# Hidden rows of a mixture of experts through DRAM and VectorE transposes instead of TensorE transposes

## The chip, the cores and the metric

The kernel runs on one core of one Trainium2 chip. The metric is the time of one execution in microseconds (us), as the device records it, with all inputs and the output in the chip's memory (DRAM). Lower is better. TensorE is called PE in the rows, VectorE DVE, ScalarE ACT, GpSimd POOL and SyncE SP.

## What is computed

Three stages follow each other: attention with a sliding window and four sink keys, a dense layer, and a mixture of eight experts. The change lies in the third stage alone, on 1536 tokens of 512 numbers:

```python
# x: 1536 x 512, w1: 8 x 512 x 1024, w2: 8 x 1024 x 512
logits = x @ w_gate
noisy_logits = logits + np.log1p(np.exp(x @ w_noise)) * noise
top2 = the two largest of each row of noisy_logits
top2_w = softmax over these two
for e in range(8):
    for k in range(2):
        mask = top2[:, k] == e
        h = np.maximum(x[mask] @ w1[e], 0.0)
        out[mask] += top2_w[mask, k, None] * (h @ w2[e])
```

All matrix products are of fp32 accuracy: an operand is split in a rounded part ("hi", in the matmul type fp32r) and the rest ("lo"), and three products (hi by hi, hi by lo, lo by hi) are summed.

## The kernel before

The five engines run programs written by hand, with an explicit semaphore for each hand-over; an engine's instructions run in the order of its code. A buffer number behind a name tells copies apart; `bank0` to `bank7` are the eight PSUM banks.

**Sorting.** After the dense layer each token's row is scattered to `sorted_x` in DRAM, grouped by expert. The experts' rows are then cut into tiles of 128 rows; there are `TILES` = 31 slots for tiles, and this input fills 29 of them (tiles 29 and 30 are computed for nothing). Tables made by VectorE (`tile_row_i`, `tile_expert_i`, `tile_slot_i`, `tile_end_i`) say where each tile's rows lie, whose expert they are, which half of the weight ring they use, and after which tile each expert ends. By the requests for weights in the trace the first six experts end behind tiles 3, 7, 10, 14, 17 and 20.

**One tile** is five steps. `turn_rows(t)`: TensorE transposes the tile's rows `xs` (4 transposes into bank 0), and ScalarE and VectorE copy them out as `xsT_hi` and `xsT_lo` (`rows_turned_out`). `up(t)`: 24 matmuls with the first matrix into banks 1 and 2. `relu_out(t)`: ScalarE and VectorE write one half each of `hid`, 128 rows by 1024. `turn_hidden(t)`: TensorE transposes `hid` (8 transposes into banks 3 and 4), and the two engines copy them out as `hidT_hi` and `hidT_lo` (`hid_turned_out`). `down(t)`: 24 matmuls with the second matrix into bank 5; VectorE copies the result to `ys` (`result_out`) and ScalarE's queue stores it to `sorted_y` in DRAM (`store_rows`).

**Order on TensorE.** The loop over tiles 3 to 29 has the order of these lines, so the second matrix lags one tile behind the first:

```python
with pe.Fori(3, TILES - 1) as t:
    up(t)
    turn_rows(t + 1)
    down(t - 1)
    turn_hidden(t)
```

**Between tiles 2 and 3** VectorE also computes the gates, ten small instructions (lines 1212 to 1220); in the changed kernel they stand behind its first two transposes, and the turned rows of tile 4 and the ReLU of tile 3 behind them.

**Weights.** The ring has two halves of 8 MB, one expert each. An expert's 4 MB come as four pieces of 1 MB into `ring_raw` (pieces 0 and 1 the first matrix, 2 and 3 the second), and GpSimd splits each in place into hi and lo (`split`, two instructions a piece). From the third expert on GpSimd's own queue requests the pieces, all four when `expert_done` says that the expert two before has ended. SyncE's queue loads the tiles' rows.

**End.** When all real tiles are stored, GpSimd gathers each token's second row (`gathered_b`, 12 indirect transfers), VectorE weighs and adds it, and SyncE stores the output.

Below are the functions that the diff touches.

## Time and profile before

| | |
|---|---|
| Time, median of 3 runs (lowest, highest) | 782.83 us (780.29, 783.93) |
| The profiled execution | 780.96 us |
| Its span, first to last instruction | 779.3 us |
| Mean granted TensorE clock, as a share of full speed | 0.991 |
| Busy share of PE, DVE, ACT, POOL | 97%, 38%, 29%, 58% |

The profile is of one execution; the times in its rows are in us from the first instruction. The device's time of that execution is 1.66 us more than the span. An engine that is busy for most of the span need not be the one that sets the end; that is read from the chain of work that ended last.

### The profile page before, as it was taken

What the parts mean: (1) busy time and instruction counts of PE and PEld (TensorE: products, weight loads), DVE (VectorE), ACT (ScalarE), POOL (GpSimd) and SP (SyncE); (2) the same over time, 40 slices, a digit from 0 to 9 for tenths busy, and PEclk for the clock granted to TensorE, in tenths of its full rate; (3) what the DMA queues carried; (4) which work ended last, traced back from release to release, by engine and by line L of the source; (5) the groups of instructions that cost most, each with busy time, mean ns of one, the idle gap of its engine ahead of it and who ended that gap; (6) DMA issues with size and microseconds to landing.
All of it is one profiled execution on the core that took longest, in us unless ns stands there. A gap on an engine that the chain in (4) does not pass through costs nothing.

```text
span 779.3 us, 13024 instructions
## 1 busy us (share of the span) xinstructions
PE 758.5 (97%) x4116; PEld 640.3 (82%) x4117; DVE 298.1 (38%) x821; ACT 225.9 (29%) x527; POOL 454.2 (58%) x264
## 2 busy tenths in 40 slices
PE   7999999999999999999999999999999999999993
PEld 5677889899989999898877888888888888888882
DVE  4777543235323522444564222223222222322225
ACT  5999522233223222322412111111111111111110
POOL 6888996000300200049699395798939898954723
PEclk8999999999999999999999999999999999999998
DMA  8642493000200100043631431617143434315228
GB/s 287 235 138 91 143 341 118 0 2 0 82 1 0 52 28 0 0 156 124 259 122 55 150 146 41 256 40 257 52 167 130 159 137 167 130 53 161 82 79 285
DMA packets 37276, 92.06 MB, mean 118 GB/s; under 512 B 5761, under 2 KB 5889, under 8 KB 37249
## 3 DMA queue, kind: packets, MB, share of 16 engines
q1 hardware_dynamic: 22416, 45.83, 16.9%
q0 software_dynamic: 10368, 37.75, 13.4%
q10 hardware_dynamic: 4464, 8.13, 2.8%
q8 instruction: 15, 0.25, 0.1%
q14 instruction: 13, 0.10, 0.0%
HBM read 67.06 MB, written 24.64 MB: 118 GB/s over the span
## 4 chain that ended last, share of the span: by engine, by line
PE 93%; DMA 2%; POOL 2%; ACT 1%; issue 1%; DVE 1%; POOLq 0%; ACTq 0%; DVEq 0%
PE bank L1465 21%; PE bank L1493 21%; PE bank L1379 17%; PE bank L1329 17%; PE bank L1282 4%; PE bank L1273 3%; PE bank L1474 3%; PE bank L1255 2%; DMA gathered_b<-sorted_y,arena 2%; PE bank L1454 2%; PE bank L1395 1%; POOL gathered_b L715 1%; PE bank L1389 1%; ACT arena L739 1%; POOL arena L643 0%
## 5 line engine op out<-in xcount | busy, mean ns | idle before, releaser
L1493 PE MATMUL bank<-ring,hidT_hi 128*128 (+1 forms) x496 | 158.4, 400 | 2.2 <-DVE hidT_lo L1114 2.2
L621 POOL TENSOR_TENSOR ring<-ring_raw,ring 128x2048 fp32r<-128x2048 f32 x32 | 148.0, 4625 | 2.5
L667 POOL DMA_INDIRECT sorted_x<-y_rows,arena x24 | 25.2, 1050 | 204.5 <-DVEq L1049 198.4
L1465 PE MATMUL bank<-ring,xsT_hi 128*128 (+1 forms) x496 | 136.0, 396 | 1.5 <-DVE xsT_lo L1096 1.5
L619 POOL TENSOR_TENSOR ring<-ring_raw,ones 128x2048 fp32r<-128x2048 f32 x32 | 115.8, 3619 | 22.1 <-DMA ring_raw<-in_moe_w 22.1
L1379 PE MATMUL bank<-w_out_sb,gated_hi 128*128 128x512 f32 x384 | 121.2, 397 | 0.0
L1493 PEld LDWEIGHTS bank<-ring,hidT_hi 128*128 128x128 f32 x496 | 90.9, 188 | 22.5 <-issue 2.7
L1465 PEld LDWEIGHTS bank<-ring,xsT_hi 128*128 128x128 f32 x496 | 90.9, 188 | 19.6 <-issue 2.2
L1493 PE MATMUL bank<-ring,hidT_lo 128*128 (+1 forms) x248 | 97.9, 395 | 0.0
L1329 PE MATMUL bank<-xT_hi,w_in_hi 128*128 (+1 forms) x256 | 86.8, 339 | 0.0
L1329 PE MATMUL bank<-xT_lo,w_in_hi 128*128 (+1 forms) x256 | 86.1, 336 | 0.0
L1329 PE MATMUL bank<-xT_hi,w_in_lo 128*128 (+1 forms) x256 | 86.0, 336 | 0.0
L1379 PEld LDWEIGHTS bank<-w_out_sb,gated_hi 128*128 128x128 f32 x384 | 71.2, 188 | 12.5
L970 DVE TENSOR_TENSOR arena<-bank,arena 128x384 f32<-128x384 f32 x64 | 35.6, 557 | 114.7 <-ACT arena L794 110.6
L854 ACT CAST hidT_hi<-bank 128x512 fp32r<-128x512 f32 x62 | 33.3, 590 | 156.8 <-PE bank L1474 156.8
L1465 PE MATMUL bank<-ring,xsT_lo 128*128 (+1 forms) x248 | 76.6, 390 | 0.0
L1379 PE MATMUL bank<-w_out_sb,gated_lo 128*128 128x512 f32 x192 | 76.0, 396 | 0.0
L794 ACT ACTIVATE arena<-bank 128x384 f32<-128x384 f32 x64 | 31.4, 491 | 138.9 <-PE bank L1329 138.9
L1108 DVE COPY ys<-bank 128x512 f32<-128x512 f32 x30 | 20.8, 692 | 122.5 <-PE bank L1493 122.5
L1101 DVE TENSOR_SCALAR hid<-bank 128x512 f32<-128x512 f32 x31 | 21.4, 691 | 114.5 <-PE bank L1465 114.5
L849 ACT ACTIVATE hid<-bank 128x512 f32<-128x512 f32 x31 | 18.5, 598 | 151.6 <-PE bank L1465 151.6
L974 DVE TENSOR_TENSOR gated_lo<-arena,gated_hi 128x384 fp32r<-128x384 f32 x64 | 44.6, 697 | 40.4 <-ACT gated_hi L799 40.4
(184 smaller groups left out, 1093.8 us busy)
## 6 DMA issues: line engine op xcount, KB each, us to landing
ring_raw<-in_moe_w POOLq DMA_DIRECT2D x24, 1024.0 KB, 9.3
ring_raw<-in_moe_w SPq DMA_DIRECT2D x8, 1024.0 KB, 6.3
xs<-sorted_x SPq DMA_DIRECT2D x31, 256.0 KB
sorted_y<-ys ACTq DMA_DIRECT2D x31, 256.0 KB
sorted_y<-zeros SPq DMA_DIRECT2D x1, 4864.0 KB, 25.1
arena<-in_k SPq DMA_DIRECT2D x8, 520.0 KB, 4.1
w_in_raw<-in_moe_w_in SPq DMA_DIRECT2D x2, 2048.0 KB, 9.4
arena<-in_q SPq DMA_DIRECT2D x8, 384.0 KB, 3.2
```

The lines of the kernel that those rows point to most:

```text
L619: pool.tensor_tensor(hi, raw, one_like(raw), ALU.mult).then_inc(rounded, 1)
L621: ins = pool.tensor_tensor(lo, raw, hi.bitcast(F32), ALU.subtract)
L667: pool.indirect_dma_start(out=sorted_x[:, :], out_offset=bass.IndirectOffsetOnAxis(ap=row_at[k][:, kk:kk + 1], axis=0), in_=y_rows_all[:, ...
L794: act.activation(tanh_h[fc % 2][:, :], bank[fc % 2][:, 0:BLK], ACT.Tanh).then_inc(tanh_ready, 1)
L854: act.copy(hidT_hi[:, half * BANK:(half + 1) * BANK], bank[3 + half][:, :]).then_inc(hidT_rounded, 1)
L970: dve.tensor_tensor(gated[fc % 2][:, :], bank[fc % 2][:, 0:BLK], tanh_h[fc % 2][:, :], ALU.subtract).then_inc(gated_ready, 1)
L974: dve.tensor_tensor(gated_lo[fc % G][:, :], gated[fc % 2][:, :], gated_hi[fc % G][:, :].bitcast(F32), ALU.subtract).then_inc(gated_split, 1)
L1282: last = pe.matmul(attn_bank[half][D * u:D * u + D, at:at + w], lhs, rhs, start=start, stop=stop, skip_group_check=True)
L1329: last = pe.matmul(bank[fc % 2][:, 0:BLK], w[:, at:at + P], x[:, bass.ds(blk * CH + c, 1), :].rearrange("p a s -> p (a s)"), start=c == 0 ...
L1379: last = pe.matmul(bank[2 + kk][:, :], g[fc % G][:, kk * P:(kk + 1) * P], w_out_sb[:, fc, w, :], start=fc == 0 and n == 0, stop=fc == FC - ...
L1465: last = pe.matmul(bank[1 + half][:, :], x[:, c * P:(c + 1) * P], ring[:, bass.ds(at * 2 * WE + (w + c * FE + half * BANK), BANK)], start= ...
L1493: last = pe.matmul(bank[5][:, :], x[:, c * P:(c + 1) * P], ring[:, bass.ds(at * 2 * WE + (w + CH * FE + c * DM), DM)], start=c == 0 and n ...
```

## The change

For tiles 2 to 30 `hid` is no longer transposed by TensorE. ScalarE's queue writes it to a DRAM tensor `hid_by_lane` (pieces of 1 KB, cut in four column blocks of 256), and reads it back into `hid_lanes`, where partition 32b + i holds rows 4i to 4i+3 of column block b (4 KB that lie together in DRAM). VectorE then transposes blocks of 32 by 32, in two instructions a tile, into the same banks 3 and 4: it reads `hid_lanes` with a step of 8 elements and writes the bank with a step of 4. What follows (`hid_turned_out`) is as before. For the hidden columns to come out in this order, the second matrix is loaded with row 8p + c in partition p, chunk c; tiles 0 and 1 are still transposed by TensorE, whose transposes therefore read `hid` with a step of 8 columns.

The second matrix now lags two tiles: while `down(t - 2)` runs, the rows of tile t travel. `up` waits in addition until banks 1 and 2 are evicted (`evicted`). The loads of tile rows move from SyncE's queue to ScalarE's from tile 4 on. SyncE's queue requests the weights from the third expert on: the first matrix once the expert two before has had its last `up`, the second once it has had its last `down`.

```diff
-        xsT_hi = place_at("xsT_hi", xsT_at, [DM], F32R)
-        xsT_lo = place_at("xsT_lo", xsT_at + DM, [DM], F32R)
+        xsT_hi = [place_at(f"xsT_hi{b}", xsT_at + 2 * b * DM, [DM], F32R) for b in range(2)]
+        xsT_lo = [place_at(f"xsT_lo{b}", xsT_at + (2 * b + 1) * DM, [DM], F32R) for b in range(2)]
...
+        hid_cols = hid[:, :].rearrange("p (r c) -> p c r", c=EC)
+        lane_blocks = hid_lanes[:, :].rearrange("p (g r c) -> p g c r", g=QUAD, c=EC)
...
+        hid_by_lane = nc.dram_tensor("hid_by_lane", (QUAD, P, FE // QUAD), F32, kind="Internal").ap()
...
-        w2_view = w2.rearrange("e (c o p) n -> p (e c) o n", o=2, p=P)
+        w2_view = w2.rearrange("e (p c o) n -> (e p) c o n", o=2, p=P)
...
+            for e in range(RING, E):
+                expert = expert_at(e)
+                last = sp.value_load(tile_end_i[0:1, e - RING:e - RING + 1], min_val=1, max_val=TILES)
+                for j, (used_up, n) in enumerate(((hid_ready, last), (hid_ready, last),
+                                                  (expert_done, last + 1), (expert_done, last + 1))):
+
+                    sp.wait_ge(used_up, n)
+                    dst, src = raw_piece(e, expert, j)
+                    sp.dma_start(dst, src).then_inc(piece_loaded[e % RING][j], 16)
...
-                    for j in range(4):
-                        dst, src = raw_piece(e, expert, j)
-                        pool.dma_start(dst, src).then_inc(piece_loaded[j], 16)
...
+            def load_rows(t):
+
+                act.wait_ge(xs_turned, t)
+                at = act.value_load(tile_row_i[0:1, bass.ds(t, 1)], min_val=0, max_val=E * CAP - P)
+                act.dma_start(xs[:, :], sorted_x[bass.ds(at, P), :]).then_inc(xs_loaded, 16)
+
+            def hid_out(t, first=False):
+
+                act.wait_ge(relu_act, t + 1)
+                act.wait_ge(relu_dve, t + 1)
+                if not first:
+
+                    act.wait_ge(hid_read, 16 * (t - 2))
+                act.dma_start(hid_by_lane.rearrange("b t q -> t b q"),
+                              hid[:, :].rearrange("t (b q) -> t b q", b=QUAD)).then_inc(hid_written, 16)
+
+            def hid_in(t, first=False):
+                act.wait_ge(hid_written, 16 * (t - 1))
+                if not first:
+
+                    act.wait_ge(hid_turned, 2 * t)
+                act.dma_start(hid_lanes[:, :], hid_by_lane.rearrange("b (i g) q -> (b i) (g q)", g=QUAD)
+                              ).then_inc(hid_read, 16)
...
+            def tile(t, load=True):
+                relu_out(t)
+                hid_out(t)
+                rows_turned_out(t + 1)
+                if load:
+                    load_rows(t + 2)
+                hid_in(t)
+                hid_turned_out(t - 1, used=t)
+                store_rows(t - 2)
...
+            def turn_hidden(t):
+
+                dve.wait_ge(hid_read, 16 * (t - 1))
+                for half in range(2):
+
+                    dve.wait_ge(hidT_ready, 2 * t - 1 + half)
+                    dve.transpose(bank[3 + half][:, :].rearrange("p (c i g) -> p g c i", c=EC // 2, g=QUAD),
+                                  lane_blocks[:, :, half * (EC // 2):(half + 1) * (EC // 2), :]).then_inc(hid_turned, 1)
...
+            def tile(t):
+                relu_out(t, written=True)
+                rows_turned_out(t + 1)
+                result_out(t - 2)
+                hid_turned_out(t - 1)
+                turn_hidden(t)
...
             pe.wait_ge(tables_ready, 1)
-            up(2)
-            turn_rows(3)
-            turn_hidden(2)
-            with pe.Fori(3, TILES - 1) as t:
-                up(t)
+            up(2, rows=3)
+            up(3, b=1, evicted=True, rows=4)
+            with pe.Fori(4, TILES - 1) as t:
+                up(t, evicted=True)
                 turn_rows(t + 1)
-                down(t - 1)
-                turn_hidden(t)
-            up(TILES - 1)
+                down(t - 2)
+            down(TILES - 3)
+            up(TILES - 1, evicted=True)
             down(TILES - 2)
-            turn_hidden(TILES - 1)
             down(TILES - 1)
```

VectorE, the loop over tiles, of before: one round is the ReLU of the right half (`hid`), the rest of the turned rows (`xsT_lo`), the result (`ys`), and the two halves of `hidT_lo`.

```order
L1231 ISA
L1101 TENSOR_SCALAR hid_86<-bank2 128x512
L1095 REGISTER_ALU
L1096 TENSOR_TENSOR xsT_lo_88<-bank0,xsT_hi_87 128x512
L1107 ISA
L1108 COPY ys_84<-bank5 128x512
L1113 ISA
L1114 TENSOR_TENSOR hidT_lo_83<-bank3,hidT_hi_82 128x512
L1113 REGISTER_ALU
L1114 TENSOR_TENSOR hidT_lo_83<-bank4,hidT_hi_82 128x512
```

The same loop of the changed kernel, from the turned rows on; the ReLU stands just ahead of these rows.

```order
L1144 TENSOR_TENSOR xsT_lo0_89<-bank0,xsT_hi0_87 128x512
L1168 COPY ys_84<-bank5 128x512
L1173 ISA
L1174 TENSOR_TENSOR hidT_lo_83<-bank3,hidT_hi_82 128x512
L1173 REGISTER_ALU
L1174 TENSOR_TENSOR hidT_lo_83<-bank4,hidT_hi_82 128x512
L1149 REGISTER_ALU
L1152 ISA
L1153 STREAM_TRANSPOSE bank3<-hid_lanes_91 128x4x128
L1153 STREAM_TRANSPOSE bank4<-hid_lanes_91 128x4x128
L1296 REGISTER_ALU
L1296 COMPARE_AND_BRANCH
```

Two transposes stand last in the round, so the next tile's ReLU stands behind them.

ScalarE, the loop over tiles, of before: ReLU of the left half, the turned rows, the two halves of `hidT_hi`, and the request to store `ys`.

```order
L849 ACTIVATE hid_86<-bank1 128x512
L844 REGISTER_ALU
L845 CAST xsT_hi_87<-bank0 128x512
L853 ISA
L854 CAST hidT_hi_82<-bank3 128x512
L853 REGISTER_ALU
L854 CAST hidT_hi_82<-bank4 128x512
L858 ISA
L858 DMA sorted_y<-ys_84 128x512
```

The same loop of the changed kernel, behind the ReLU and up to the first half of `hidT_hi`.

```order
L860 DMA hid_by_lane<-hid_86 128x4x256
L844 REGISTER_ALU
L845 CAST xsT_hi0_87<-bank0 128x512
L850 ISA
L850 TENSOR_LOAD arena_75
L850 ISA x2
L851 ISA
L851 DMA xs_85<-sorted_x 128x512
L864 ISA
L867 REGISTER_ALU
L868 DMA hid_lanes_91<-hid_by_lane 128x1024
L880 ISA
```

Three requests have come in between: the write of `hid`, the load of the rows of tile t + 2, and the read into `hid_lanes`, which waits for the write and stands ahead of the copies to `hidT_hi`.

## Rows read from the trace of the kernel before

**Rows 1.** The page: span, then busy time, share and instructions of each engine.

```profile
span 779.3 us, 13024 instructions
...
PE 758.5 (97%) x4116; PEld 640.3 (82%) x4117; DVE 298.1 (38%) x821; ACT 225.9 (29%) x527; POOL 454.2 (58%) x264
```

**Rows 2.** The chain that ended last, from 390 us: start, length, what.

```profile
405.84 5.46 PE bank L1465 x24
...
411.32 0.60 ACT hid L849
...
414.04 5.74 PE bank L1465 x24
...
426.67 5.48 PE bank L1465 x24
432.15 0.44 PE bank L1454 x4
432.59 5.60 PE bank L1493 x24
438.19 0.88 PE bank L1474 x8
...
637.27 5.71 PE bank L1465 x24
...
736.60 5.47 PE bank L1465 x24
742.07 0.44 PE bank L1454 x4
742.50 5.60 PE bank L1493 x24
...
749.17 2.04 DMA sorted_y<-ys
...
751.97 0.99 POOL gathered_b L715
...
776.13 0.75 DVE gathered_a L1239
```

**Rows 3.** Two tiles' stretches: busy by engine, clock, DMA share, GB/s.

```profile
426.67:439.06 12.39, 12.39 (x62) 10.23 (x61) 3.36 (x5) 2.15 (x5) 2.80 (x2) 1.00 0.14 42
439.06:451.46 12.40, 12.40 (x62) 10.23 (x61) 3.37 (x5) 2.15 (x5) 8.32 (x6) 1.00 0.88 323
```

**Rows 4.** Groups by line: busy us, mean ns, idle before.

```profile
L1114 DVE TENSOR_TENSOR hidT_lo<-bank,hidT_hi 128x512 fp32r<-128x512 f32 x62 | 39.9, 686 | 8.1 <-ACT hidT_hi L854 7.7 <-issue 0.4
...
L1474 PE MATMUL bank<-ident,hid 128*128 128x128 f32 x248 | 32.2, 273 | 0.3 <-ACT hid L849 0.3
...
L621 POOL TENSOR_TENSOR w_out_sb<-w_out_raw,w_out_sb 128x512 fp32r<-128x512 f32 x16 | 21.7, 1354 | 1.3
...
L1101 DVE TENSOR_SCALAR hid<-bank 128x512 f32<-128x512 f32 x31 | 21.4, 691 | 114.5 <-PE bank L1465 114.5
```

**Rows 5.** DMA issues: count, KB each, median us from issue to landing.

```profile
ring_raw<-in_moe_w POOLq DMA_DIRECT2D x24, 1024.0 KB, 9.3
...
arena<-in_k SPq DMA_DIRECT2D x8, 520.0 KB, 4.1
...
arena<-in_q SPq DMA_DIRECT2D x8, 384.0 KB, 3.2
```

**Rows 6.** VectorE in order of time, the gates behind tile 2, first and last.

```profile
414.49 0.16 DVE L1212 TENSOR_SCALAR bank<-arena 128x12 f32<-128x12 f32 x1
...
416.02 0.17 DVE L1220 TENSOR_TENSOR arena<-arena,bank 128x12 f32<-128x12 f32 x1
```

**Rows 7.** GpSimd in order of time: request of the seventh expert, splits of its first matrix.

```profile
614.94 2.97 POOL L696 DMA_DIRECT2D ring_raw<-in_moe_w  x4
620.47 3.60 POOL L619 TENSOR_TENSOR ring<-ring_raw,ones 128x2048 fp32r<-128x2048 f32 x1 [2.56 <-DMA ring_raw<-in_moe_w]
...
632.39 4.61 POOL L621 TENSOR_TENSOR ring<-ring_raw,ring 128x2048 fp32r<-128x2048 f32 x1
```

More of the change, by code:

```diff
@@ L436, in raw_piece @@
             else:
[L437 removed]
+                src = w2_view[bass.ds(expert * P, P), :, j - 2, :]
             return piece(ring_raw[e % RING], j), src
@@ L555, in _ @@
             sp.wait_ge(tile_rows_known, 1)
-            with sp.Fori(2, TILES) as t:
-                start = tile_start(t)
-                sp.wait_ge(scattered, 16 * TOP * TT)
+            sp.wait_ge(scattered, 16 * TOP * TT)
+            for t in (2, 3):
                 sp.wait_ge(xs_turned, t)
-                load_rows(start)
+                load_rows(sp.value_load(tile_row_i[0:1, t:t + 1], min_val=0, max_val=E * CAP - P))
+            sp.wait_ge(tables_ready, 1)
+            for e in range(RING, E):
[6 more added lines that the diff above has]
+                    sp.dma_start(dst, src).then_inc(piece_loaded[e % RING][j], 16)
             for i in range(TT):
@@ L849, in relu_out, with hid_turned_out @@
                 act.activation(hid[:, 0:BANK], bank[1][:, :], ACT.Relu).then_inc(relu_act, 1)
-            def hid_turned_out(t):
+            def hid_turned_out(t, used=None):
+                if used is not None:
+                    act.wait_ge(expert_done, used)
                 for half in range(2):
@@ L870, in _ @@
             act.activation(gate_e[:, :], gate_d[:, :], ACT.Exp).then_inc(route_act, 1)
-            def tile(t, more):
-                relu_out(t)
-                if more:
-                    rows_turned_out(t + 1)
-                hid_turned_out(t)
-                store_rows(t - 1)
             relu_out(1)
@@ L883, in _ @@
             store_rows(1)
+            rows_turned_out(3, 1)
+            act.wait_ge(tile_rows_known, 1)
+            act.wait_ge(scattered, 16 * TOP * TT)
+            load_rows(4)
             relu_out(2)
-            rows_turned_out(3)
-            hid_turned_out(2)
-            with act.Fori(3, TILES - 1) as t:
-                tile(t, True)
-            tile(TILES - 1, False)
+            hid_out(2, first=True)
+            hid_in(2, first=True)
+            rows_turned_out(4)
+            load_rows(5)
+            relu_out(3)
+            hid_out(3)
+            hid_turned_out(2, used=3)
+            hid_in(3)
+            def tile(t, load=True):
[7 more added lines that the diff above has]
+                store_rows(t - 2)
+            with act.Fori(4, TILES - 2) as t:
+                tile(t)
+            tile(TILES - 2, load=False)
+            store_rows(TILES - 3)
+            hid_turned_out(TILES - 2, used=TILES - 1)
+            relu_out(TILES - 1)
+            hid_out(TILES - 1)
+            hid_in(TILES - 1)
+            hid_turned_out(TILES - 1, used=TILES)
+            store_rows(TILES - 2)
             act.wait_ge(expert_done, TILES + 1)
@@ L1205, in _ @@
             result_out(1)
+            rows_turned_out(3, 1)
             relu_out(2)
-            rows_turned_out(3)
-            hid_turned_out(2)
+            turn_hidden(2)
             dve.wait_ge(route_act, 3 * NBLK + 1)
@@ L1221, in _ @@
             dve.sem_inc(gates_ready, 1)
-            def tile(t, more):
-                relu_out(t)
-                if more:
-                    rows_turned_out(t + 1)
-                result_out(t - 1)
-                hid_turned_out(t)
-            with dve.Fori(3, TILES - 1) as t:
-                tile(t, True)
-            tile(TILES - 1, False)
+            rows_turned_out(4)
+            relu_out(3, written=True)
+            hid_turned_out(2)
+            turn_hidden(3)
+            def tile(t):
[4 more added lines that the diff above has]
+                turn_hidden(t)
+            with dve.Fori(4, TILES - 1) as t:
+                tile(t)
+            result_out(TILES - 3)
+            hid_turned_out(TILES - 2)
+            relu_out(TILES - 1, written=True)
+            turn_hidden(TILES - 1)
+            result_out(TILES - 2)
+            hid_turned_out(TILES - 1)
             for i in range(TT):
@@ L1461, in up @@
                 pe.wait_ge(xsT_ready, t + 1)
+                if evicted:
+                    pe.wait_ge(relu_act, t)
+                    pe.wait_ge(relu_dve, t)
                 for c in range(CH):
-                    for n, (x, w) in enumerate(((xsT_hi, 0), (xsT_hi, WE), (xsT_lo, 0))):
+                    if rows is not None and c == CH // 2:
+                        turn_rows(rows)
+                    for n, (x, w) in enumerate(((xsT_hi[b], 0), (xsT_hi[b], WE), (xsT_lo[b], 0))):
                         for half in range(2):
```

48 lines of the change are left out of this document (21 added, 27 removed).

## The prediction, on record before the changed kernel ran

> **What bounds the kernel now.** I read the page first. TensorE is busy for 97% of the span, and the next, GpSimd, for 58% [rows 1]. Then the chain that ended last, in order of time, from tile 2 to the end [rows 2]. From 426.67 us it is TensorE alone: `up` 5.48 us, `turn_rows` 0.44, `down` 5.60, `turn_hidden` 0.88, and then the next `up` at 439.06, without a gap. The two tile stretches say the same: PE is busy for all of 12.39 us, while VectorE works 3.36 and ScalarE 2.15, at full clock, whether no weights travel (42 GB/s) or four pieces do (323 GB/s) [rows 3]. So a tile costs what TensorE is given, and the other engines have over 8 us to spare in each. The second thing to see is the end: the chain leaves TensorE when `down(28)`, begun at 742.50, is done; its result is stored, the gathers begin at 751.97, and the rest of the 779.3 us is gathers and stores [rows 2]. Tiles 29 and 30 run beside them.
>
> **The sum** is made in the span of the profiled execution, 779.3 us.
>
> *TensorE's transposes.* From the start of `up(4)` at 426.67 to the end of `up(29)` at 742.07 there are 25 whole tiles and one `up` [rows 2]. Each whole tile loses its 8 transposes, 0.88 us: 12.39 becomes 11.51. That is 25 x 0.88 = **-22.0 us**, if nothing else is late.
>
> *What must hide.* The rows now take this way: ReLU, ScalarE's request, write to DRAM, ScalarE's request, read back, two VectorE transposes, and only then VectorE's next ReLU, which stands behind them in its program. This is a ring of one round per tile, so a tile can't be shorter than the ring. Its parts:
> - ReLU 0.69 [rows 4].
> - The write of 512 KB. Below: the 256 KB store of `ys` landed in 2.04 us [rows 2]. Above: 520 KB of keys in 4.1 [rows 5], which shared the queues with other loads. I take 3.2, between them, since pieces of 1 KB to DRAM have no row.
> - The read of 512 KB. Below: 384 KB in 3.2; above again 4.1 [rows 5]. I take 3.8, by size.
> - The two transposes. The trace has none. Below: 0.65 each, as the other 128x512 instructions of VectorE, which run at 0.686 and overlap a little; above: 1.35, GpSimd's subtraction of that size [rows 4]. No step of 8 elements in a big VectorE instruction is in the trace either. I take 0.65, since the work is one pass over as many elements, so 1.3.
> - Three hand-overs of 0.1.
>
> That is 0.69 + 3.2 + 3.8 + 1.3 + 0.3 = 9.3 us against 11.51, with bounds 7.5 (2.04 + 3.2 + 1.3 + 1.0) and 11.9 (4.1 + 4.1 + 2.7 + 1.0). Moreover the ReLU may end up to some 5.3 us after `up` without TensorE noticing, as `turn_rows` and `down` (6.04) come before the next `up`, and `xsT_lo` (0.69) stands behind the ReLU; it now ends 0.7 after. So 4.6 us of lateness can be borrowed. The work itself has room: VectorE 3.36 + 1.3 = 4.7 of 11.51, ScalarE 2.15 and four requests, of about 0.4 each.
>
> *The Trainium skill* (DMA: Bandwidth & Descriptors, section "Anatomy of one DMA") gives 2.0 us and bytes/436e3 for a transfer on GpSimd's path, so 3.2 us for each leg by estimate. The ring would be 8.7 and the start below 0.6 shorter. No row here has a lone 512 KB transfer.
>
> *Weights.* The requests leave GpSimd (2.97 us per expert [rows 7]) and come apart: the first matrix about a tile earlier, the second about one later. Each pair of pieces is 2 MB, 6 us at 323 GB/s [rows 3], beside the write or the read. If it doubles a leg, each costs 3 to 4 us of the ring; two per expert make up to 7, against 3 to 4 tiles with 2.2 us to spare in each, and 4.6 borrowed. I take 0. GpSimd itself was at its limit once: it requested the seventh expert at 614.94, split the first matrix from 620.47 to 637.00 [rows 7], and the `up` that needs it ran from 637.27 for 5.71 instead of 5.48 [rows 2]. Now, with `up(4)` at 424.7, `up(14)` ends at 545 and `down(14)` at 574, which releases the sixth expert's second matrix; it lands 6 us later and is split by 597, and the seventh's first matrix, long loaded, is split by 613; `up(21)` wants it at 620. So 7 us to spare, and no wait.
>
> *The start.* `up(2)` starts at 405.84 as before and holds the 4 transposes of the rows: it ends at 411.75. `up(3)` must now wait for the ReLU: 412.5, and ends with its own 0.44 at 418.4. `down(2)` no longer fills the time behind it, and `up(4)` waits for VectorE: 412.5 + 7.3 (legs and hand-overs) = 419.8, transposes 421.1, the gates, 1.7 us from 414.49 to 416.19 [rows 6], 422.8, `xsT_lo` and ReLU 424.2; the second request of weights falls in the read, +0.5: 424.7. Before it was 426.67. The work of `down(2)` and `turn_hidden(3)` is thus displaced, not lost: **-2.0 us**. With legs of 5.2 in all it would be -3.8, with the upper bounds +0.6.
>
> *The end.* `down(28)` used to follow `up(29)` by 0.44. Now `down(27)` is between, 5.60, and since `hidT` is one buffer, `down(28)` also waits for ScalarE's and VectorE's first half: 0.6 + 0.7 + 0.1 = 1.4. **+7.0 us**. What queues behind on VectorE, `result_out(28)`, stands behind `turn_hidden(29)`, which by the ring ends 3 us before `down(28)`.
>
> *Gathers* now share the DMA engines with the write and read of tile 30, 1 MB against 6 MB of gathers and stores: **+0.5 us** (0 to 2). TensorE's 16 transposes with a step of 8, tiles 0 and 1: 0 to 1.8 (twice their 0.88 each), mostly beside other waits; I take 0.
>
> Sum: -22.0 - 2.0 + 7.0 + 0.5 = -16.5. Span 762.8, its own time 764.5 instead of 780.96. The median before is 1.87 us above that execution, so I take the difference from the median: 782.83 - 16.5 = **766.3 us**, -2.1%.
>
> **Rivals.** A measurement of this kernel can hardly tell 0.5%, 3.9 us, from no change: 778.9 to 786.7.
>
> - *The ring is a little short of hidden* (0.15): bursts of weights or legs of 4.1 us use up the borrowed 4.6, and TensorE waits a few us at each of six experts. With 1 to 2 us each, 772 to 779.
> - *The gain is eaten* (0.10): 779 to 787. It needs a ring of about 12.2 us: 25 x (12.2 - 11.5) + 2.9 at the start - 4.6 borrowed = 16.
> - *The legs through DRAM are slow and the kernel gets slower* (0.10): the write and read together over 9.9 us instead of 7.0. At 10.7 the ring is 13.0: 766.3 + 25 x 1.5 + 3.7 - 4.6 = 803. For it: 1 KB pieces, the weights, two transfers of rows on the same queue. Against: 42 GB/s in most stretches [rows 3], and 4.1 us for 520 KB with neighbours.
> - *The transposes are slow* (0.08): over 2.1 us each, the ring again passes 12.2. At 2.4 each it is 12.8: 766.3 + 32 + 3.5 - 4.6 = 797. For it only the steps of 8 read and 4 written; against it, no row of VectorE above GpSimd's 1.35 us for this size. The Trainium skill (SBUF — State Buffer, section "Door 1") says that each access to a new 16-byte line pays, and that PSUM's lines have 8 bytes; these steps leave the line at each element. It gives no price for VectorE.
>
> **How the numbers follow.** The forecast, 761 to 772, has 0.57. Below it the shortest ring gives -1.8 more at the start, the gathers may cost nothing (-0.5), and the medians scatter by 2 to 3: low 761. Above, I go through the eaten gain and the edge of the slower cases: high 789, which leaves out the worst of them. Faster is the forecast and the first rival, 0.72; same 0.10; slower 0.18.
>
> **What would show it.** `turn_hidden`'s pieces gone from the chain, and tiles of 11.51 us on TensorE. The transposes near 0.65 us each, the write and read near 3.2 and 3.8. `up(4)` starting 12.2 us after `up(3)` did, behind a wait for VectorE's ReLU. A wait of 1.4 us ahead of `down(28)`, and gathers from about 735. GpSimd idle more often, for weights. If instead each `up` waits for VectorE's ReLU and VectorE for `hid_lanes`, the ring is the bound and I am wrong; if TensorE waits for `ring`, it is the weights.

## The result, and the profile after

The changed kernel took 789.26 us (median of 7 runs, 786.34 to 792.28) against 783.59 for the kernel before (median of 7, 780.29 to 784.06): the ratio is 1.0079, with a 95% interval from 1.0056 to 1.0103. It is slower by 0.8%, where 2.1% less was forecast. The profiled execution took 789.29 us, its span is 787.4.

The page of the changed kernel, with the rows that answer to [rows 1, 4, 5]:

```profile
span 787.4 us, 12786 instructions
...
PE 746.5 (95%) x3884; PEld 624.8 (79%) x3885; DVE 358.1 (45%) x879; ACT 229.1 (29%) x528; POOL 436.4 (55%) x240
...
L1153 DVE STREAM_TRANSPOSE bank<-hid_lanes 128x512 f32<-128x512 f32 x58 | 64.0, 1148 | 44.5 <-DMA hid_lanes<-hid_by_lane 44.5
...
ring_raw<-in_moe_w SPq DMA_DIRECT2D x32, 1024.0 KB, 8.4
hid_by_lane<-hid ACTq DMA_DIRECT2D x29, 512.0 KB, 3.1
hid_lanes<-hid_by_lane ACTq DMA_DIRECT2D x29, 512.0 KB, 3.4
```

TensorE is busy for 12 us less than before, although 29 tiles no longer have their transposes of 0.88 us: matmuls that run slower behind pauses, below, take the rest. The median write and read are as fast as assumed. But the span is 8 us longer: TensorE stands still for some 20 us more. The chain that ended last shows where (start, length, what):

```profile
412.80 3.25 DMA hid_by_lane<-hid
416.07 3.42 DMA hid_lanes<-hid_by_lane
419.51 2.10 DVE bank L1153 x2
...
424.89 8.50 PE bank L1542 x24
433.39 0.44 PE bank L1524 x4
433.83 5.59 PE bank L1571 x24
439.43 5.44 PE bank L1542 x24
...
450.90 5.44 PE bank L1542 x24
...
468.81 8.63 DMA hid_by_lane<-hid
...
504.85 10.37 DMA hid_by_lane<-hid
515.32 0.33 ACTq L868
...
519.53 7.40 PE bank L1571 x24
...
592.12 11.22 DMA hid_by_lane<-hid
...
721.76 5.46 PE bank L1542 x24
...
747.06 7.39 PE bank L1571 x24
```

The tile from 439.43 to 450.90 takes 11.47 us, as forecast (12.39 in [rows 2, 3]). Then, at five of the six loads of a first matrix, the chain leaves TensorE for a *write* of `hid` that takes 8.5 to 11.2 us; with nothing else under way a write takes 2.9 to 3.3 (two more slow ones, 8.54 at 556.32 and 10.28 at 632.19, aren't shown). Behind each TensorE starts late, and where it stood still longest the next 24 matmuls take 7.4 us instead of 5.6. What is asked for around the write at 504.85, in order of time, first on SyncE's queue (two views, the second a part of the first), then on ScalarE:

```profile
498.59 6.44 SPq L577 DMA_DIRECT2D ring_raw<-in_moe_w  x4
...
504.05 0.99 SPq L577 DMA_DIRECT2D ring_raw<-in_moe_w  x2
```

```profile
503.90 0.60 ACT L873 ACTIVATE hid<-bank 128x512 f32<-128x512 f32 x1 [4.29 <-PE bank L1542]
504.85 0.38 ACTq L860 DMA_DIRECT2D hid_by_lane<-hid  x1
...
515.32 0.33 ACTq L868 DMA_DIRECT2D hid_lanes<-hid_by_lane  x1
515.77 0.59 ACT L881 CAST hidT_hi<-bank 128x512 fp32r<-128x512 f32 x1 [9.85 <-DMA hid_by_lane<-hid]
```

The end of an expert's last `up` releases both the request for the next first matrix (2 MB, at 504.05) and, one ReLU later, the write (at 504.85). Of the four requests in the first row, the two at 498.59 and 499.35 are the second matrix of the expert before; it landed only at 509.86. So this write has 4 MB beside it. It is the same at the writes of 11.22 and 10.28 us. At the two of 8.63 and 8.54 us only the 2 MB of the first matrix were under way, and at the one load that is left, the first in time (419.52), the write came 5.2 us behind the request and took 3.75. ScalarE can ask for the read only when the write has landed, and the copies to `hidT_hi`, which the next `down` needs and which have nothing to do with this transfer, stand behind that request. The waits of the whole span (us in total, times, longest):

```profile
ACT hidT_hi L881 <- DMA hid_by_lane<-hid: 57.8, 9, 10.7
...
PE bank L1571 <- DVE hidT_lo L1174: 13.7, 6, 7.3
```

ScalarE's wait is this large in total. But of TensorE's 13.7 us for `hidT_lo` only 3.0, in three waits, fall between 430 and 725 us, where the collisions are; the rest is at the end of the kernel. So the late copies alone don't explain the loss.

There is a second victim. ScalarE's load of the next tile's rows, asked for at 506.19, lands just as late (median 2.8 us, longest 10.7). TensorE in order of time:

```profile
516.74 0.66 PE L1524 MATMUL bank<-ident,xs 128*128 128x128 f32 x4 [1.41 <-DMA xs<-sorted_x]
519.53 1.22 PE L1571 MATMUL bank<-ring,hidT_hi 128*128 x2 [2.14 <-issue]
```

`turn_rows` waits 1.41 us for `xs`, and the `down` behind it starts 2.14 later, though its first half of `hidT_lo` was done at 517.07. What fills the 2.14 us is in TensorE's own program: between `turn_rows` and `down` it reads two registers (lines 1557 and 1558, the tile's expert and its half of the ring). Such a read took 0.30 to 1.18 us. In a quiet tile both are done while `up` still runs; here they stand behind the wait for `xs`, at 516.85 and 518.47. So it is at all five collisions:

| `xs` landed | first half of `hidT_lo` done | `down` starts |
|---|---|---|
| 478.03 | 479.29 | 480.47 |
| 516.69 | 517.08 | 519.53 |
| 565.44 | 566.72 | 567.71 |
| 604.13 | 605.19 | 606.90 |
| 643.05 | 644.32 | 645.51 |

`down` starts 1.0 to 2.5 us after its data are there and 2.3 to 2.8 us after `xs` has landed, so `xs` with the two reads behind it is what releases it. The matmuls themselves stood still for `xs` at three of the five (1.41, 1.57 and 0.43 us). The share of each victim is an estimate: at the three big collisions TensorE stood still for 9.4 us, and with `xs` on time the copies alone would have left some 5 of it, from the end of an undisturbed `turn_rows` to the time in the second column. At the two small ones (0.73 and 0.47 us ahead of `down`) they would have left nothing; there some 0.3 and 0.4 us came ahead of the next `up` as well, by the way that was forecast: write, read, transposes, VectorE's ReLU.

Four stretches with the columns of [rows 3]; first the tile of `up(4)` and a quiet one, then the wait and the `down` behind it:

```profile
424.89:439.43 14.54, 14.54 (x53) 11.66 (x54) 4.85 (x6) 2.26 (x4) 14.38 (x5) 0.80 0.46 167
439.43:450.90 11.47, 11.47 (x53) 9.38 (x53) 5.58 (x7) 2.26 (x4) 6.64 (x2) 1.00 0.48 158
...
510.00:519.53 9.53, 5.99 (x28) 4.51 (x27) 2.04 (x4) 1.64 (x3) 9.37 (x4) 1.00 0.83 304
519.53:526.93 7.40, 7.40 (x25) 5.95 (x26) 3.29 (x4) 0.59 (x1) 7.40 (x2) 0.77 0.43 122
```

The clock granted to TensorE is 0.80 and 0.77 in the stretches that follow a pause, so it stood at the lower level, 1.2 GHz, for part of them; before the first of the two TensorE had been idle for 5.57 us (from 419.32), before the other for 1.41 and 2.14.

### The profile page after: what moved, and what is told of

Its sections match the earlier page's. It is cut to its first block, busy times and chain, and to the rows that moved or that the text cites. A ratio compares the mean times of both kernels' runs of the same rounds, so it can differ in the third digit from the quotient of the medians.

```text
span 787.4 us, 12786 instructions
## 1 busy us (share of the span) xinstructions
PE 746.5 (95%) x3884; PEld 624.8 (79%) x3885; DVE 358.1 (45%) x879; ACT 229.1 (29%) x528; POOL 436.4 (55%) x240
## 4 chain that ended last, share of the span: by engine, by line
PE 80%; DMA 11%; DVE 3%; issue 2%; ACT 2%; POOL 1%; ACTq 0%; DVEq 0%; POOLq 0%
PE bank L1449 17%; PE bank L1399 17%; PE bank L1542 17%; PE bank L1571 16%; DMA hid_by_lane<-hid 8%; PE bank L1352 4%; PE bank L1343 3%; DMA hid_lanes<-hid_by_lane 3%; PE bank L1325 2%; PE bank L1465 1%; DVE bank L1153 1%; DVE hid L1161 1%; PE bank L1524 1%; PE bank L1459 1%; ACT arena L739 1%
## 5 line engine op out<-in xcount | busy, mean ns | idle before, releaser
L1571 PE MATMUL bank<-ring,hidT_hi 128*128 (+1 forms) x496 | 165.1, 415 | 17.9 <-DVE hidT_lo L1174 13.7
L1571 PEld LDWEIGHTS bank<-ring,hidT_hi 128*128 128x128 f32 x496 | 95.3, 197 | 41.4 <-issue 20.0
L1542 PEld LDWEIGHTS bank<-ring,xsT_hi 128*128 128x128 f32 x496 | 94.0, 191 | 29.2 <-issue 9.5
L1571 PE MATMUL bank<-ring,hidT_lo 128*128 (+1 forms) x248 | 101.2, 408 | 0.0
L1153 DVE STREAM_TRANSPOSE bank<-hid_lanes 128x512 f32<-128x512 f32 x58 | 64.0, 1148 | 44.5 <-DMA hid_lanes<-hid_by_lane 44.5
L1571 PEld LDWEIGHTS bank<-ring,hidT_lo 128*128 128x128 f32 x248 | 48.7, 197 | 12.0
L1174 DVE TENSOR_TENSOR hidT_lo<-bank,hidT_hi 128x512 fp32r<-128x512 f32 x62 | 39.9, 685 | 33.9 <-ACT hidT_hi L881 33.7
```

The lines of the kernel that those rows point to most:

```text
L1153: dve.transpose(bank[3 + half][:, :].rearrange("p (c i g) -> p g c i", c=EC // 2, g=QUAD), lane_blocks[:, :, half * (EC // 2):(half + 1) * ...
L1174: dve.tensor_tensor(hidT_lo[:, cols], bank[3 + half][:, :], hidT_hi[:, cols].bitcast(F32), ALU.subtract).then_inc(hidT_ready, 1)
L1542: last = pe.matmul(bank[1 + half][:, :], x[:, c * P:(c + 1) * P], ring[:, bass.ds(at * 2 * WE + (w + c * FE + half * BANK), BANK)], start= ...
L1571: last = pe.matmul(bank[5][:, :], x[:, c * P:(c + 1) * P], ring[:, bass.ds(at * 2 * WE + (w + CH * FE + c * DM), DM)], start=c == 0 and n ...
```

## The experiments

**Theory A**: the first matrix's burst meets the write, ScalarE's program makes `down` start late by it, and a late restart costs 2 to 3 us more at the lower clock. No expectation speaks of the load of `xs` in the same burst, and no run moves it alone. **Rivals**: it is the ring as a whole that is too long (slow transposes, slow legs), or the order in ScalarE's program alone. Each diff is against the changed kernel, where no other is named. Each time is a median, each ratio is to the kernel before, which had medians of 781.86 to 782.84 us beside these runs.

### No weights on the way

```diff
-            for e in range(RING, E):
-                ...
-                    sp.dma_start(dst, src).then_inc(piece_loaded[e % RING][j], 16)
...
+                    pool.wait_ge(hid_ready, last + 1)
+                    pool.sem_inc(up_split, 1)
+                    pool.wait_ge(expert_done, last + 2)
+                    pool.sem_inc(down_split, 1)
```

It leaves out the loads and splits of the weights from the third expert on.

> This kernel leaves out the loads and the splits of all experts' weights from the third on (they compute with the first two experts' weights); the rest is as in the changed kernel. Theory A, the write of hid is slow only beside the load of a first matrix: every write takes about 3.1 us as the median one does, no `up` or `down` waits behind `up(4)`, and the time falls by what the tiles from 4 to 28 took over 11.48 us each beyond the slow restart, 18 us, to about 771. Rival B, the way of the rows through DRAM is too long by itself for some tiles, whatever else travels: waits stay and the time is above 783.

Measured: 772.22 us, ratio 0.9874 (0.9855 to 0.9892). Writes and reads between tiles 4 and 27 never stand on the chain; what is left are the first restart (`up(4)` 7.12 us) and the end. So the ring in itself is short enough, the rival "the whole ring is too long" falls, and the 16 to 17 us (by the ratios, by the medians) come from the weights. By this run alone that could also be their splits; the next one moves only a request.

### The first matrix requested after the write

```diff
-                for j, (used_up, n) in enumerate(((hid_ready, last), (hid_ready, last),
+                for j, (used_up, n) in enumerate(((moved, last), (moved, last),
...
                 act.wait_ge(hid_written, 16 * (t - 1))
+                act.sem_inc(moved, 1)
```

> SyncE requests an expert's first matrix only once the write of hid of the last tile that used it has landed, about 4 us later than now. Theory A: the four writes of 8.6 to 11.2 us fall to near 3.5, the reads behind them lengthen from 3.4 to some 6 to 8, but nothing on ScalarE waits for a read, so the `down`s no longer wait; about 772 (768 to 778). Rival B: 787 to 790, since the same bytes travel in the same tile. Rival D, the weights become late for GpSimd: TensorE waits for the ring, over 790.

Measured: 771.48 us, ratio 0.9868 (0.9846 to 0.9889): with all the work done it is as fast as without weights. ScalarE and, below, SyncE and VectorE in order of time, for the expert that had the write of 11.22 us:

```profile
584.17 0.38 ACTq L861 DMA_DIRECT2D hid_by_lane<-hid  x1
...
588.66 0.39 ACTq L870 DMA_DIRECT2D hid_lanes<-hid_by_lane  x1
589.32 1.08 ACT L883 CAST hidT_hi<-bank 128x512 fp32r<-128x512 f32 x2 [4.01 <-PE bank L1574]
```

```profile
588.71 0.96 SPq L578 DMA_DIRECT2D ring_raw<-in_moe_w  x2
```

```profile
593.82 2.24 DVE L1156 STREAM_TRANSPOSE bank<-hid_lanes 128x512 f32<-128x512 f32 x2 [2.59 <-DMA hid_lanes<-hid_by_lane]
```

The same burst now starts with the read (0.05 us behind its request), and the read is through in 5.0 us (588.66, and the transposes begin at 593.82). Nothing on ScalarE stands behind the read, and VectorE has the time. The copies wait for TensorE's `down`, as they should. The load of `xs`, asked for at 585.54, is ahead of the burst too, so this edit cures both victims and doesn't weigh them apart.

### The first matrix requested after the read

The same with `moved` counted by VectorE when it has waited for the read.

```diff
                 dve.wait_ge(hid_read, 16 * (t - 1))
+                dve.sem_inc(moved, 1)
```

> SyncE requests an expert's first matrix only once the read into hid_lanes of the last tile that used it has landed, some 7.5 us later than now. Theory A: the burst now falls between a read and the next write, of which it may touch the start; writes of at most 5 us, about 770 (767 to 776), equal to or a little better than after the write. Rival B: no change, 787 to 790. Rival D: weights late, over 790.

Measured: 782.56 us (772.51 to 787.76 in ten runs, the widest spread here), ratio 0.9961 (0.9924 to 0.9998), a miss by 12. The burst of 7 to 8 us, moved 5 us later, reaches into the next tile's write. The chain that ended last:

```profile
516.87 6.56 DMA hid_by_lane<-hid
...
533.61 7.04 DMA hid_lanes<-hid_by_lane
...
617.70 7.64 DMA hid_lanes<-hid_by_lane
```

Of the writes behind a first matrix those on the chain take 6.2 to 6.8 us; reads that are requested 0.8 to 1.3 us behind a second matrix take 7.0 to 7.6. The ring's spare time is gone and stays gone. Apart isn't enough; the burst must end before the next write.

### The read requested behind the copies

```diff
-                hid_in(t)
                 hid_turned_out(t - 1, used=t)
                 store_rows(t - 2)
+                hid_in(t)
```

> ScalarE requests the read into hid_lanes behind the copies to hidT_hi and the store, so its wait for the write no longer stands ahead of them; the weights are requested as in the changed kernel. If the order on ScalarE turns slow writes into waits of `down` (13.7 us of TensorE's waits were for hidT_lo), the waits for hidT_lo go away, but the reads of all tiles start later (7.2 us behind `up` instead of 4) and a write of 10 us still makes the next ReLU late: a part of the 18 us comes back, 776 to 783. If the order does not matter, 787 to 790. If the later reads make the ring too long for all tiles, over 792.

Measured: 793.85 us, ratio 1.0128 (1.0093 to 1.0163). The copies no longer wait, but every read starts later, behind TensorE's `down`, and VectorE waits for it in each round:

```profile
DVE bank L1153 <- DMA hid_lanes<-hid_by_lane: 135.3, 29, 8.5
```

In the changed kernel this wait is 44.5 us in 21. The third of the expected outcomes came, a ring too long for all tiles. So the order in ScalarE's program can't simply be turned: the read's early request is what hides the ring. What the order costs beside the weights this run doesn't show, since it lengthens every tile.

### The weights requested 0.6 us behind the write

As the kernel with `moved` after the write, but counted just behind the write's request.

```diff
                               hid[:, :].rearrange("t (b q) -> t b q", b=QUAD)).then_inc(hid_written, 16)
+                act.sem_inc(moved, 1)
...
                 act.wait_ge(hid_written, 16 * (t - 1))
-                act.sem_inc(moved, 1)
```

> SyncE requests an expert's first matrix once the write of hid of the last tile that used it has been requested (not landed), about 1 us later than in the changed kernel; write and load then run beside each other, the write's bytes first in line. Theory A1, a write behind 2 MB of weights waits for all of them (first come, first served on the DMA engines): writes of at most 5 us and the time of w1_after_write, 769 to 775. Theory A2, the DMA engines take turns between the queues, whoever was first: writes still of 6 to 8 us beside the weights, and a time between, 777 to 786.

Measured: 782.81 us, ratio 1.0010 (0.9986 to 1.0035). The time is the one of theory A2, but most of the writes are those of A1. At the loads behind tiles 3, 7, 14 and 20 the write takes 3.5, 3.4, 3.5 and 4.6 us, where in the changed kernel those of tiles 7, 14 and 20 took 8.6, 8.5 and 10.3. So to be first by 0.6 us did protect the write. Only at tiles 10 and 17 it doesn't: 8.8 us (505.99) and 10.1 (589.83, landed by 600.01). There, as at tile 20, the second matrix of the expert before, requested 6.3 us ahead of the write, was still under way. What is asked for behind the weights now pays in the write's place, the read and `xs`:

```profile
554.49 3.45 DMA hid_by_lane<-hid
...
558.04 8.21 DMA hid_lanes<-hid_by_lane
...
591.17 10.62 DMA xs<-sorted_x
```

### Pieces of 4 KB in the write

`hid` goes out in whole rows of 4 KB, and four requests read it back in pieces of 1 KB.

```diff
-                act.dma_start(hid_by_lane.rearrange("b t q -> t b q"),
-                              hid[:, :].rearrange("t (b q) -> t b q", b=QUAD)).then_inc(hid_written, 16)
+                act.dma_start(hid_by_lane[:, :], hid[:, :]).then_inc(hid_written, 16)
...
+                for b in range(QUAD):
+                    act.dma_start(hid_lanes[32 * b:32 * b + 32, :].rearrange("i (g q) -> i g q", g=QUAD),
+                                  hid_by_lane.rearrange("(i g) (b q) -> b i g q", g=QUAD, b=QUAD)[b]
+                                  ).then_inc(hid_read, 16)
```

> The changed kernel with another layout in DRAM: hid is written as whole rows, in pieces of 4 KB, and read back by four requests in pieces of 1 KB; the weights are requested as in the changed kernel. If the write is slow beside the weights because its pieces are small (1 KB against 4 KB of theirs, in turn), it falls from 8.6 to 11.2 us to about 5, and the time to 772 to 778. If it is slow because it stands behind the bytes that are already under way, it stays at 8 or more, and the time at 786 to 794.

Measured: 813.84 us, ratio 1.0384 (1.0336 to 1.0432). A lone write is shorter, 2.63 us; behind a first matrix it takes 4.9 to 8.2, so neither expectation holds as a whole. The moments have moved too: the longest was asked for 1.2 us behind the weights, the others 3 us or more. The time says nothing of the write: the four requests take ScalarE 0.62 us each (median), and the slowest reads beside weights 7.1 to 8.2.

### Pieces of 2 KB and 1 KB in the weights

Two requests of half the columns each, or four of a quarter, for a first matrix; GpSimd waits for all of them.

```diff
+                    if j < 2:
+                        w = FE // 4
+                        for part in range(2 * j, 2 * j + 2):
+                            dst = ring_raw[e % RING][:, 0:2 * PIECE].rearrange("p (c n) -> p c n", c=CH)[:, :, part * w:(part + 1) * w]
+                            src = w1_view[:, bass.ds(expert * CH, CH), part * w:(part + 1) * w]
+                            sp.dma_start(dst, src).then_inc(piece_loaded[e % RING][j], 16)
+                        continue
```

> The changed kernel, but SyncE's two requests for a first matrix take half the columns of all four chunks each, so that their pieces are 2 KB instead of 4 KB; bytes, number and moment of the requests stay. GpSimd waits for both before it splits. Turns by pieces (the write's 512 pieces of 1 KB and the weights' pieces are served alternately, in equal numbers): a lone write is 3.1 us, about 1.4 and 0.5 MB at 300 GB/s; beside 4 KB pieces it ends with all 2.5 MB, 1.4 + 8.3 = 9.7 (8.5 to 11.2 was seen), beside 2 KB pieces when 1.5 MB are through: 1.4 + 5.0 = 6.4 us. Then no `down` is late, the 18 us come back, and the time is 769 to 774. Rival, what is asked first is served first or the bytes alone count: the five writes stay at 8.5 to 11.2 us and the time at 785 to 792.

> As the 2 KB kernel, with four requests of a quarter of the columns each, so pieces of 1 KB. Turns by pieces: the write ends when 1 MB is through, 1.4 + 3.3 = 4.8 us; the weights have 2048 pieces and may themselves take longer than 8.4 us, which GpSimd's splits can bear by some us. Time 769 to 774, as with 2 KB, or up to 3 more if the splits come late. Rival, as before: writes of 8.5 to 11.2 us and 785 to 792.

Measured: 785.04 us, ratio 1.0045 (1.0016 to 1.0073), and 784.01 us, ratio 1.0031 (1.0005 to 1.0056). From the chain of the kernel with 2 KB:

```profile
469.95 8.04 DMA hid_by_lane<-hid
...
505.26 9.25 DMA hid_by_lane<-hid
...
554.54 7.58 DMA hid_by_lane<-hid
```

The five writes have a mean of 8.7 us with 2 KB (7.6 to 9.5) and 8.3 with 1 KB (7.6 to 8.5), against 9.8 in the changed kernel; 6.4 and 4.8 were forecast. Whether the times are better than the changed kernel's isn't clear, since the intervals of the ratios overlap or touch.

The trace also has the start of each piece, and it shows what the forecast left out. With nothing else under way, the first piece of the write starts 0.9 to 1.2 us behind its request. At the five slow writes of the changed kernel it starts 3.6 to 4.0 us behind it, with 1 KB pieces in the weights 3.7 to 4.2. From then on the two queues do take turns by number: from 474 to 475 us the changed kernel started 65 pieces of the write and 70 of the weights (of 4 KB), and from 474.9 to 475.9 the kernel with 1 KB pieces 171 and 200. So turns by number of pieces hold once the write has begun; the 3 us ahead of its first piece, in which only weights move, are what the sum of 4.8 lacked. In the kernel where the write was asked for 0.6 us ahead of the weights, its first piece at tiles 3, 7 and 14 started after 0.9 us, as if alone.

### The order at the start

On the kernel with `moved` after the write. VectorE's ReLU of tile 3 no longer waits behind the transposes of tile 2 and the gates.

```diff
             relu_out(2)
+            rows_turned_out(4)
+            relu_out(3, written=True)
             turn_hidden(2)
+            hid_turned_out(2)
...
-            rows_turned_out(4)
-            relu_out(3, written=True)
-            hid_turned_out(2)
             turn_hidden(3)
```

> On top of w1_after_write (771.5 us), VectorE turns out the rows of tile 4 and does the ReLU of tile 3 ahead of its first two transposes and the gates, not behind them. Theory A says that `up(4)` waits 6.9 us only because VectorE sits in the wait for the first read, and then runs 7.8 us instead of 5.5 at a lower clock: both go away, up(4) starts within 1 us of the end of `up(3)`, and the time falls by 7 to 9 us, to about 763. If the rows' first way through DRAM is the bound instead, the wait moves to `down(2)` and the time stays at 770 to 772.

Measured: 763.67 us, ratio 0.9742 (0.9698 to 0.9787). The chain: `up(3)`, ReLU, `up(4)`.

```profile
419.66 2.79 PE bank L1545 x12
...
422.47 0.70 DVE hid L1164
...
423.42 5.73 PE bank L1545 x24
```

A pause of 1.0 us instead of 7.00 in the kernel it was made from, and `up(4)` takes 5.73 instead of 7.75. (In this execution `up(3)` waited for a split of GpSimd's and started 3 us later than in the other, so the span, 766.7, is longer than the median would have it.)

### Matmuls that keep the clock up

Also on the kernel with `moved` after the write: 27 matmuls into the unused bank 5 fill the pause ahead of `up(4)`.

```diff
             up(3, b=1, evicted=True, rows=4)
+            pe.wait_ge(ys_ready, 2)
+            for _ in range(27):
+                pe.matmul(bank[5][:, :], xsT_hi[1][:, 0:P], xsT_hi[1][:, :], start=True, stop=True)
```

> On top of w1_after_write, TensorE runs 27 matmuls of no use (their result is overwritten) while it waits ahead of up(4), some 6.2 us of work in a wait of 6.9. If the lower clock comes from the idle stretch, `up(4)` takes 5.5 instead of 7.8 us and the time falls by 2.3 us to about 769. If the slow matmuls have another cause, such as a transfer that slows their operands, up(4) stays at 7.8 and the time at 771.

Measured: 769.88 us, ratio 0.9843 (0.9788 to 0.9897). In its chain `up(4)` starts behind as long a wait but takes 5.74 us; without the filler, in the kernel it was made from, 7.75:

```profile
420.92 6.12 PE bank L1602 x27
...
427.13 5.74 PE bank L1545 x24
```

So the 2 us are the clock's and not a wait inside `up`. The time, 1.6 us less, can't be told from 771.48.

### Transposes without steps

Again on the kernel with `moved` after the write: VectorE reads and writes with a step of 1, so the rows come out in another order and the output differs.

```diff
-        lane_blocks = hid_lanes[:, :].rearrange("p (g r c) -> p g c r", g=QUAD, c=EC)
+        lane_blocks = hid_lanes[:, :].rearrange("p (g c r) -> p g c r", g=QUAD, c=EC)
...
-                    dve.transpose(bank[3 + half][:, :].rearrange("p (c i g) -> p g c i", c=EC // 2, g=QUAD),
+                    dve.transpose(bank[3 + half][:, :].rearrange("p (g c i) -> p g c i", c=EC // 2, g=QUAD),
```

> On top of w1_after_write, the two VectorE transposes read and write with a step of 1 (the output is then in another order, so this computes something else). If the steps of 8 and 4 cost the time above a plain 128x512 instruction, a transpose falls from 1.15 to about 0.65 us; if it is the transpose itself, it stays near 1.15.

Measured, in one execution: 770.5 us, so no difference in time that one run could show, but the row of the page is

```profile
L1156 DVE STREAM_TRANSPOSE bank<-hid_lanes 128x512 f32<-128x512 f32 x58 | 38.2, 704 | 42.1 <-DMA hid_lanes<-hid_by_lane 38.5 <-issue 3.7
```

0.70 us each, 1.15 with the steps. The rival "slow transposes", over 2.1 us each, had fallen with the 1.15 already.

### Both edits and a shorter end

The write first, the new order at the start, and tile 30 transposed by TensorE as in the kernel before.

```diff
             relu_out(TILES - 1)
-            hid_out(TILES - 1)
-            hid_in(TILES - 1)
...
             down(TILES - 2)
+            turn_hidden(TILES - 1)
             down(TILES - 1)
```

> w1_after_write and start_order together, and tile 30, whose rows no token needs, is transposed by TensorE as before the change, without the way through DRAM. start_order gave 763.7 us. There down(30) waited 8.1 us and ran 8.2 instead of 5.6, and the sums of the last stage stood behind tile 30's transposes on VectorE until 752.7 us though the gathers had begun at 736.9. If these sums set the end, it falls by 3 to 5 us, to 759 to 761; if the gathers and stores of the output do, it stays at 763 to 764.

Measured: 761.84 us, ratio 0.9727 (0.9705 to 0.9749), the lowest median here, 2.7% below the kernel before. That the third edit adds to the first two isn't shown (763.67 without it, and the runs overlap). The end of its chain:

```profile
725.19 7.42 PE bank L1571 x24
...
752.40 6.99 DMA gathered_b<-sorted_y,arena
```

`down(28)` still starts behind a pause of 2.93 us, and the gathers set the end again, as in [rows 2].

## Why the prediction was wrong

The step that failed is in the part on weights: "If it doubles a leg, each costs 3 to 4 us of the ring; two per expert make up to 7 [...] I take 0." It priced the meeting of weights and rows at nothing; it cost 18.3 us. Five things of it didn't hold.

- *The size.* The leg triples, from 3.1 to 8.5 to 11.2 us: it ends about when the weights do (their median is 8.4).
- *Two bursts, not one.* I wrote that the requests "come apart". At the experts of three tiles they come together: the second matrix of one expert is requested 5.5 us ahead of the next expert's first, and lands 9.2 to 11.6 us behind its request. These are the three writes of 10.3 to 11.2 us.
- *The moment.* I laid the bursts at some place "beside the write or the read". In the program it is fixed: SyncE's request and the write have the same releaser, so at five of the six the first matrix is requested 0.8 us ahead of a write, and all five stood on the chain. At the first one VectorE's ReLU was late, and the write came 5.2 us behind.
- *Who waits.* I let the lateness be borrowed on VectorE's side, from the ring. On that way TensorE stood still for only 0.3 and 0.4 us, at two of the experts. ScalarE is stopped: its wait for the write stands ahead of `hidT_hi`, and `down` needs that. And TensorE is stopped, in `turn_rows`, for `xs`, whose load the change put into the same burst; its two register reads and `down` stand behind that wait. My own rows of the order showed it; I named the three requests and not what is queued behind the wait, nor the load as one that the weights can delay.
- *The restart.* I priced no pause but its own length. Three `down` at 7.4 us cost 1.8 each on top.

Together: from the start of `up(4)` to that of `up(28)` are 296.9 us, where 24 x 11.48 = 275.5 were due. 3.1 of the 21.4 are the first `up`, 18.3 the collisions. The five cost 1.6, 5.5, 1.4, 5.6 and 4.2 us. The experiments show both terms: with the request moved 17.8 us come back (789.26 to 771.48; 16.5 by the two ratios), and the order at the start gives 7.8 more. How much of the 18.3 is ScalarE's stop and how much is `xs` is estimated from one trace, not shown: no run moves one without the other.

The other terms, by their numbers:

- *Tiles of 11.51*: 11.47 where nothing collides. Right.
- *`up(4)` at 424.7*: 424.89, right, by errors that cancel: the transposes took 2.10 us for both instead of 1.3, the legs 3.25 and 3.42 instead of 7.0. What was missing is the length of `up(4)`, 8.50 instead of 5.5: **+3.1**. The 1.8 us gained at its start (2.0 were forecast) are a loss of 1.2 at its end.
- *Transposes 0.65 each*: 1.15. It adds 1.0 to the ring and nothing to the time, since the ring is hidden; the steps cost 0.45 us each. That steps cost is what the Trainium skill (SBUF — State Buffer, section "Door 1") let expect; by these rows the trace agrees.
- *Write 3.2, read 3.8*: 3.1 and 3.4 (medians of all 29). By the Trainium skill (DMA: Bandwidth & Descriptors, section "Anatomy of one DMA") it is 3.2 for both by estimate; the lone transfers agree, though its path is another queue's.
- *The end, +7.0*: the order and the wait ahead of `down(28)` are there, and `up(28)` to the end of `down(28)` took 32.7 us instead of 30.0. 1.8 of the difference is again the lower clock (7.39 at 747.06, behind a pause of 2.35), the rest a longer wait, beside gathers (write 4.29 at 729.55).
- *Gathers +0.5*: from the end of `down(28)` to the end of the span 32.95 us, 31.2 before, so +1.8. Within my bounds.
- *GpSimd and SyncE not late*: right; TensorE never waits for `ring`.

0.2 + 20.6 (21.4, less 24 x 0.03) + 2.7 + 1.3 make 24.8; between 762.8 and 787.4 lie 24.6, and the difference is rounding.

The mechanism on which the gain rested was right. With the request moved and the start reordered the kernel is at 763.67, near the 766.3 of the forecast; that it isn't there as it stands comes from when one request is released. Of the rivals, "the ring is a little short of hidden" is nearest in mechanism: it has TensorE wait at each of six experts for the bursts of weights. It priced each at 1 to 2 us, where five cost 1.4 to 5.6. "The gain is eaten" is nearest in its number, but for another reason: its ring of 12.2 us in each of 25 tiles didn't come, quiet tiles had 11.48.

**What sets a slow leg, and what stays open.** The order of the requests does. A write behind 2 MB of weights took 8.5 and 8.6 us when it was requested 0.8 us after them, 6.2 to 6.8 us when 3.0 to 3.3 us after, and 3.75 when 5.2 us after: each time it has landed about 9 to 10 us after the first of those requests. Ahead of the same 2 MB, by 0.6 us, it took 3.4 to 3.5. It is so for the reads: 4.5 to 5.1 us when requested 0.05 us ahead of the burst, 6.5 to 8.2 when 0.8 to 4.1 us behind one. The Trainium skill (DMA: Bandwidth & Descriptors, section "Queues, rings and completion order") says that each DMA engine takes turns between its queues packet by packet. From the write's first piece on, the trace agrees, with about as many pieces of one queue as of the other. The 3.6 to 4.2 us ahead of that piece it doesn't account for. How many pieces a packet holds isn't seen in these traces. So it stays open why the first piece comes so late behind another queue's request, and why, beside 4 MB, being first by 0.6 us helped at tile 20 (4.6 us) and not at tiles 10 and 17 (8.8 and 10.1).

## What to carry to other kernels

When a transfer comes onto the path, look up what is released by the same event on the other queues, and in which order. Price a leg that is requested behind a big load at the sum of both sizes, not at its own; here one requested ahead of it paid almost nothing. Then read down the program of every engine that waits for a transfer of the burst, TensorE's too: the work queued behind the wait, down to the register reads, is what comes late. A big prefetch belongs behind the last of the short transfers that something waits for, where it has time to end before the next one.

## What the runs showed of the hardware

- 512 KB to DRAM took 2.9 to 3.3 us with nothing else under way. It took 8.5 and 8.6 beside 2 MB requested 0.8 us earlier on another queue, 10.3 to 11.2 where a further 2 MB had been requested some 6 us earlier, and 3.4 to 3.5 when the 2 MB were requested 0.6 us later (three times, with nothing else under way).
- Behind such a request the write's first piece started after 3.6 to 4.0 us instead of 0.9 to 1.2. After that the two queues started about as many pieces each, 65 of 1 KB to 70 of 4 KB in a microsecond.
- A register read from SBUF on TensorE's program took 0.30 to 1.18 us. Two of them with what stands around them held `down` back for 2.3 to 2.8 us behind a late wait, and for nothing where the program ran ahead.
- Behind a pause of 5.57 us 24 matmuls took 8.50 us instead of 5.44, behind one of 2.35 us 7.39 instead of 5.60, behind one of 1.63 us 5.86 and behind 0.99 us 5.73. With matmuls in the pause it was 5.74.
- A 32x32 block transpose of 128x512 from SBUF to PSUM on VectorE took 0.70 us with steps of 1, and 1.15 with a step of 8 read and 4 written.
- A request of 128 KB in pieces of 1 KB, read from DRAM, held ScalarE for 0.62 us (median), one of 512 KB in 4 KB pieces for 0.33, and one of 512 KB in 1 KB pieces written to DRAM for 0.38.
